# Range checks from the first load, the flag ahead of the last copies, and GpSimd's weight sums ahead of a wait

## The reference

```python
def _attn_ref(q, k, v, alpha):
    state = zeros((B, H, D, D))                      # B, H, S, D = 2, 8, 768, 48
    for t in range(S):
        state = alpha[:, :, t, :, None] * state + einsum('bhd,bhe->bhde', k[:, :, t], v[:, :, t])
        y[:, :, t] = einsum('bhd,bhde->bhe', q[:, :, t], state)
    return y

x = y as 1536 x 384
rms = sqrt(mean(x * x, axis=-1, keepdims=True) + 1e-06)
xn = x / rms * rms_g
g = xn @ w_gate                                      # 384 x 1536
x = (g / (1 + exp(-g)) * (xn @ w_val)) @ w_out
p = domain_probs / (domain_probs.sum(-1, keepdims=True) + 1e-09)
out = sum(p[:, e:e + 1] * (maximum(x @ w1[e], 0.0) @ w2[e]) for e in range(4))
```

## Time and profile before

| what | value |
|---|---|
| time, median of 3 runs | 701.38 us (701.12 to 702.0) |
| profiled execution, its own time | 698.92 us |
| its span in the profile | 697.2 us |
| PE busy | 683.6 us (98%) |
| DVE, ACT, POOL busy | 466.2, 265.3, 329.1 us |
| granted PE clock, mean | 1.0 |
| DMA moved | 35.14 MB |

### The profile page before, as it was taken

One profiled execution on the slowest core, in us unless ns is written; L12 is line 12 of the kernel. 1 busy time (PEld: TensorE's weight loads), 2 busy tenths in 40 slices (PEclk: granted clock), 3 DMA queues, 4 the chain that ended last, 5 costly groups with the idle time before them and its releaser, 6 DMA issues.

```text
span 697.2 us, 10727 instructions
## 1 busy us (share of the span) xinstructions
PE 683.6 (98%) x3989; PEld 633.9 (91%) x3989; DVE 466.2 (67%) x819; ACT 265.3 (38%) x482; POOL 329.1 (47%) x416
## 2 busy tenths in 40 slices
PE   7899999999999999999989999999999999999998
PEld 6699999999999999998979999999999999999997
DVE  6876657555556543216968777977797778767875
ACT  3932333222522243227534343433344334443430
POOL 3469761111111115770396586457645775577200
PEclk9999999999999999999999999999999999999999
DMA  8995380005102001000011100111011101100003
GB/s 183 225 182 116 98 170 0 9 1 103 35 1 77 1 2 44 3 0 24 1 46 46 47 23 24 46 46 38 9 46 45 46 2 46 46 24 1 23 1 136
DMA packets 71749, 35.14 MB, mean 50 GB/s; under 512 B 53904, under 2 KB 70672, under 8 KB 71696
## 3 DMA queue, kind: packets, MB, share of 16 engines
q1 hardware_dynamic: 71696, 34.44, 19.6%
HBM read 31.48 MB, written 2.36 MB: 49 GB/s over the span
## 4 chain that ended last, share of the span: by engine, by line
PE 88%; DVE 4%; SPq 3%; POOL 2%; ACT 1%; issue 1%; DMA 1%; DVEq 0%; POOLq 0%
PE out_ps L1370 12%; PE out_ps L1372 12%; PE out_ps L1371 12%; PE hid_ps L1363 7%; PE hid_ps L1365 6%; PE hid_ps L1364 6%; PE at_ps L1608 4%; PE at_ps L1607 4%; PE at_ps L1606 4%; PE hid_ps L1607 2%; PE hid_ps L1608 2%; PE hid_ps L1606 2%; SPq L460 2%; PE at_ps L1444 2%; PE at_ps L1458 1%; PE at_ps L1490 1%
## 5 line engine op out<-in xcount | busy, mean ns | idle before, releaser
L1249 DVE SCALAR_TENSOR_TENSOR x<-out_ps,prob,x 128x384 f32<-128x384 f32 x180 | 110.3, 613 | 58.2 <-PE out_ps L1372 58.2
L1371 PE MATMUL out_ps<-early_r,late_r 128*128 128x384 f32 x384 | 129.4, 337 | 0.0
L1370 PE MATMUL out_ps<-early_r,late_r 128*128 128x384 f32 x384 | 129.0, 336 | 0.4 <-DVE x L1249 0.4
L1372 PE MATMUL out_ps<-early_r,late_r 128*128 128x384 f32 x384 | 129.3, 337 | 0.0
L680 POOL TENSOR_TENSOR hid_lo<-act_sb,hid_hi 128x384 fp32r<-128x384 f32 x44 | 44.9, 1020 | 160.9 <-ACT hid_hi L891 160.9
L941 ACT COPY late<-at_ps 128x512 f32<-128x512 f32 x105 | 61.9, 589 | 103.8 <-PE at_ps L1608 100.8
L1215 DVE TENSOR_TENSOR act_sb<-hid_ps,act_sb 128x384 f32<-128x384 f32 x48 | 26.6, 555 | 79.6 <-PE hid_ps L1365 70.2
L1370 PEld LDWEIGHTS out_ps<-early_r,late_r 128*128 128x128 f32 x384 | 72.1, 188 | 6.6 <-DVE x L1249 0.9
L1371 PEld LDWEIGHTS out_ps<-early_r,late_r 128*128 128x128 f32 x384 | 72.0, 188 | 5.6
L1372 PEld LDWEIGHTS out_ps<-early_r,late_r 128*128 128x128 f32 x384 | 72.1, 188 | 0.0
L699 POOL TENSOR_TENSOR early<-stage 128x128 f32<-128x128 f32 x15 | 7.0, 470 | 126.4 <-PE at_ps L1608 98.8
(11 more groups left out here) (286 smaller groups left out, 1621.5 us busy)
## 6 DMA issues: line engine op xcount, KB each, us to landing
stage<-in_moe_w_dram SPq DMA_DIRECT2D x32, 384.0 KB, 3.5
alpha_all<-in_alpha_dram SPq DMA_DIRECT2D x8, 288.0 KB, 6.2
stage<-in_moe_w_out_dram SPq DMA_DIRECT2D x4, 576.0 KB, 4.0
out_dram<-x SPq DMA_DIRECT2D x12, 192.0 KB, 1.9
stage<-in_moe_w_gate_dram SPq DMA_DIRECT2D x8, 216.0 KB, 3.9
stage<-in_moe_w_val_dram SPq DMA_DIRECT2D x8, 216.0 KB, 4.0
a_tm<-in_alpha_dram SPq DMA_DIRECT2D x9, 192.0 KB, 4.2
k_tm<-in_k_dram SPq DMA_DIRECT2D x9, 192.0 KB, 3.7
```

The lines of the kernel that those rows point to most:

```text
L1249: dve.scalar_tensor_tensor(out=a, in0=part, scalar=p, in1=a, op0=ALU.mult, op1=ALU.add).then_inc(s_acc, 1)
L1370: pe.matmul(dst, ah, bh, start=first, stop=False)
L1371: pe.matmul(dst, ah, bl, start=False, stop=False)
L1372: return pe.matmul(dst, al, bh, start=False, stop=last)
```

## The change

1. Alpha is checked from other sources. The first quarter's two halves are checked from a_tm, where they are loaded for the attention anyway; only six parts are loaded to alpha_all: parts 2 and 3, the second quarter, in a new form (four runs for each partition), and parts 4 to 7, the second batch. CHECKED gives the order of the checks. As a_tm must keep its values until it has been checked, the clamped first quarter goes to a_first, which lies where woh will be; POOL's first split of an out piece waits until the transposes have read it. next_a waits for clamps and checks as well.
2. gcol's four DMAs are issued by ACT at its start instead of by SP.
3. FIRST has a new order: the checks stand earlier on ACT; y of the third pair is copied by ACT instead of DVE ("Y 2" for "YD 2"); the flag ("W") stands ahead of the last y and of its copies, and DVE reads the flag there ("ND"). The eight keep-warm matmuls of step "W" are gone. High and low parts and products of x go in the order FIRST_ORDER, in which the block copied last stands last; the square on DVE has a semaphore of its own (s_sqd); the counts that the engines wait for follow (not shown in the diff below).
4. In later quarters "SS" stands one place later.
5. sum_first of pair 2 no longer waits for s_vl and s_plain; sum_upper does.
6. In the last pair the first add_up stands ahead of the last split_bank.

```diff
@@ -96,6 +96,7 @@
         APARTS = 8
+        CHECKED = (0, 1, 4, 5, 6, 7, 2, 3)
         AW = B * H * S * D // P // APARTS
@@ -127,6 +128,10 @@
         wvl = sb("wvl", [P, KT, FF], F32R, reg_b)
+        reg_a_cl = ExitStack()
+        a_first = sb("a_first", [P, NCH, H * LANE], stack=reg_a_cl)
+        reg_a_cl.close()
+        assert NCH * H * LANE <= FT * DM
         woh = sb("woh", [P, FT, DM], F32R, reg_b)
...
@@ -398,7 +404,7 @@
         AT[STEP * NP].append(("N", 0))
-        AT.setdefault(STEP * NP + 2, []).append(("SS", 0))
+        AT.setdefault(STEP * NP + 3, []).append(("SS", 0))
         AT.setdefault(STEP * NP + 4, []).append(("R", 0))
@@ -406,12 +412,13 @@
                  (step.split() for step in ("F 10", "C 0", "T 0", "T 1", "TK 0", "TQ 0", "TK 1", "TQ 1", "F 5", "M 0",
-                                            "M 1", "S 0", "KS 0", "E 0", "C 1", "S 1", "KS 1", "T 2", "E 1", "KV 0",
-                                            "ST 0", "KV 1", "T 3", "ST 1", "E 2", "TK 2", "TQ 2", "Y 0", "TK 3",
-                                            "TQ 3", "E 3", "M 2", "M 3", "Y 1", "S 2", "KS 2", "E 4", "S 3", "KS 3",
-                                            "E 5", "KV 2", "ST 2", "KV 3", "ST 3", "E 6", "YD 2", "E 7", "SQ 1",
-                                            "YD 3", "SQ 2", "W 0", "SQD 3", "N 0", "XS 0", "SS 0", "R 0"))]
+                                            "M 1", "E 0", "S 0", "KS 0", "E 1", "C 1", "S 1", "KS 1", "E 2", "T 2",
+                                            "KV 0", "ST 0", "KV 1", "E 3", "T 3", "ST 1", "E 4", "TK 2", "TQ 2",
+                                            "Y 0", "TK 3", "TQ 3", "E 5", "M 2", "M 3", "Y 1", "S 2", "KS 2", "E 6",
+                                            "S 3", "KS 3", "E 7", "KV 2", "ST 2", "KV 3", "ST 3", "SQ 1", "Y 2",
+                                            "W 0", "SQ 2", "ND 0", "YD 3", "SQD 3", "N 0", "XS 0", "SS 0", "R 0"))]
         assert NP == 4
+        FIRST_ORDER = [PAIR_ORDER[f] for f in range(1, NP)]
@@ -486,6 +493,8 @@
                 sp.wait_ge(s_ta, NP * i)
+                sp.wait_ge(s_clamp, i + 1)
+                sp.wait_ge(s_sqa, 2)
                 load_quarter(i, 0)
@@ -499,28 +508,31 @@
             def load_alphas(c):
-                flat = alpha.rearrange("b h (x t) d -> (b h x) (t d)", x=P // BH)
-                sp.dma_start(alpha_all[:, c, :], flat[:, c * AW:(c + 1) * AW]).then_inc(s_all[c], 16)
+                if c < 4:
+                    hs = slice((c - 2) * H // 2, (c - 1) * H // 2)
+                    src = alpha[0, hs, TQ:2 * TQ, :].rearrange("h (p t) d -> p h (t d)", p=P)
+                    sp.dma_start(alpha_all[:, c - 2, :].rearrange("p (h x) -> p h x", h=H // 2), src
+                                 ).then_inc(s_all[c], 16)
+                else:
+                    flat = alpha[1].rearrange("h (x t) d -> (h x) (t d)", x=P // H)
+                    sp.dma_start(alpha_all[:, c - 2, :], flat[:, (c - 4) * AW:(c - 3) * AW]).then_inc(s_all[c], 16)
...
                 load_quarter(0, which, H // 2, H, s_half[which])
-            for which in (0, 1, 2):
-                load_quarter(0, which, 0, H // 2)
-                if which == 0:
-                    load_alphas(0)
-            load_alphas(1)
-            load_alphas(2)
-            load_quarter(0, 3, 0, H // 2)
-            load_alphas(3)
+            load_quarter(0, 0, 0, H // 2)
             load_alphas(4)
-            load_piece(0)
+            load_quarter(0, 1, 0, H // 2)
+            load_quarter(0, 2, 0, H // 2)
             load_alphas(5)
             load_alphas(6)
+            load_quarter(0, 3, 0, H // 2)
             load_alphas(7)
+            load_alphas(2)
+            load_piece(0)
+            load_alphas(3)
             load_piece(1)
-            rows_to_lanes(sp, gcol[:, :].rearrange("p (j n) -> p j n", n=1), rms_g.rearrange("(r n) -> r n", n=1),
-                          s_small, True)
             fill_holes(0)
...
@@ -688,10 +701,7 @@
                 w, u, _ = weight_sums(pair)
-                if pair == PLAIN + 1:
-                    pool.wait_ge(s_vl, len(V_SUMS))
-                    pool.wait_ge(s_plain, 6 * PLAIN)
-                elif pair > PLAIN + 1:
+                if pair > PLAIN + 1:
                     pool.wait_ge(s_mul, 15 * (pair - PLAIN - 1))
@@ -715,6 +725,9 @@
                 c, raw, done = pair % 2, raw_1(pair), 3 * (pair - PLAIN)
+                if pair == PLAIN + 1:
+                    pool.wait_ge(s_plain, 6 * PLAIN)
+                    pool.wait_ge(s_vl, len(V_SUMS))
                 pool.wait_ge(s_us, done + 3)
@@ -791,11 +804,18 @@
-                part = alpha_all[:, c, :]
+                part = alpha_all[:, (CHECKED[c] - 2) % APARTS, :]
                 if c == 0:
                     act.wait_ge(s_const, CONST_BIAS)
-                act.wait_ge(s_all[c], 16)
-                act.activation(part, part, ACT.Square, bias=consts[:, 1:2]).then_inc(s_sqa, 1)
+                if c < 2:
+                    half = slice(0, H // 2 * LANE) if c else slice(H // 2 * LANE, H * LANE)
+                    act.wait_ge(s_qka[0] if c else s_half[0], 16 * NCH)
+                    act.activation(part.rearrange("p (c h x) -> p c h x", c=NCH, x=D),
+                                   a_tm[:, :, half].rearrange("p c (h x) -> p c h x", x=LANE)[:, :, :, 0:D],
+                                   ACT.Square, bias=consts[:, 1:2]).then_inc(s_sqa, 1)
+                else:
+                    act.wait_ge(s_all[CHECKED[c]], 16)
+                    act.activation(part, part, ACT.Square, bias=consts[:, 1:2]).then_inc(s_sqa, 1)
                 act.wait_ge(s_sqa, c + 1)
@@ -803,15 +823,15 @@
+            act.wait_ge(s_const, CONST_T)
+            rows_to_lanes(act, gcol[:, :].rearrange("p (j n) -> p j n", n=1), rms_g.rearrange("(r n) -> r n", n=1),
+                          s_small, True)
             for name, i, f in events():
...
                 elif name == "SQ":
-                    if f == 2:
-                        act.wait_ge(s_yd, 2)
-                    else:
-                        act.wait_ge(s_yc, 2 * f + 2)
+                    act.wait_ge(s_yc, 2 * f + 2)
                     act.wait_ge(s_hole, 96)
...
@@ -1057,14 +1081,15 @@
-                    part = a_tm[:, :, :]
+                    part = held = a_tm[:, :, :]
                     if i == 0:
-                        part = a_tm[:, :, 0:H // 2 * LANE] if f else a_tm[:, :, H // 2 * LANE:]
+                        half = slice(0, H // 2 * LANE) if f else slice(H // 2 * LANE, H * LANE)
+                        part, held = a_tm[:, :, half], a_first[:, :, half]
                     if i == 0 and f == 0:
...
                         dve.wait_ge(s_qka[0], 16 * NCH * (i + 1))
-                    dve.tensor_scalar(part, part, MID - HALF, MID + HALF, ALU.max, ALU.min).then_inc(s_clamp, 1)
+                    dve.tensor_scalar(held, part, MID - HALF, MID + HALF, ALU.max, ALU.min).then_inc(s_clamp, 1)
                 elif name == "T":
...
@@ -1150,12 +1175,11 @@
                                           ).then_inc(s_wild, 1)
-                elif name == "N":
-                    if i == 0:
-                        dve.wait_ge(s_wild, 1)
-                        with dve.If(dve.value_load(wild[0:1, 0:1])):
-                            attention_by_steps()
-                        continue
+                elif name == "ND":
+                    dve.wait_ge(s_wild, 1)
+                    with dve.If(dve.value_load(wild[0:1, 0:1])):
+                        attention_by_steps()
+                elif name == "N" and i:
                     dve.wait_ge(s_sq, 2 * KT * (i + 1))
...
@@ -1347,8 +1371,11 @@
                     add_up(pair - 1, 11)
+                else:
+                    add_up(pair, 0)
                 split_bank("B", 0, 1)
-                add_up(pair, 0)
+                if pair < NPAIR - 1:
+                    add_up(pair, 0)
                 add_up(pair, 1)
...
@@ -1492,36 +1521,37 @@
                 elif name == "W":
-                    pe.wait_ge(s_st, NCH * NP)
-                    keep_warm(2)
                     pe.wait_ge(s_const, CONST_ALL)
...
                               ).then_inc(s_exsum, 1)
-                    keep_warm(6)
                 elif name == "SS":
...
                         pe.wait_ge(s_sqsum, i)
+                        mm = pe.matmul(at_ps[1][:, :], ones[:, :], x_nrm[:, 0, :], start=True, stop=True)
                     else:
-                        pe.wait_ge(s_sq, 2 * KT)
-                    for j in range(1 if i else KT):
-                        mm = pe.matmul(at_ps[1][:, :], ones[:, :], x_nrm[:, j, :], start=j == 0,
-                                       stop=j == (0 if i else KT - 1))
+                        for n, j in enumerate(FIRST_ORDER):
+                            if n == 0:
+                                pe.wait_ge(s_sq, 2 * KT)
```

(4 more changed lines are left out.)

36 lines of the change are left out of this document (22 added, 14 removed).

## The result

The changed kernel takes 694.44 us (694.12 to 695.21, 4 runs), the kernel before 701.25 beside it (700.11 to 702.0, 4 runs): ratio 0.9912 with an interval of 0.9891 to 0.9933. The profiled execution tells another story: 694.60 with a span of 692.9, against 698.92 and 697.2 before. That is 4.3 us less, close to the sum of 4.1. So the sum of the terms held and the step from the profiled execution to the median did not.

The account below looks back on a forecast made before the run. The prediction took TensorE (PE) as the bound, with 88% of the chain that ended last. Its terms, 1.7 + 0.2 + 1.75 + 0.45 = 4.1 us, came off the median 701.38, giving 697.3, range 695.8 to 699.3.

Parts of the forecast that it names:

- edit 4: Pair 2: POOL's sums done in its idle time remove PE's 1.84 us stop; 1.75 us gained, bounds 1.4 to 2.2.
- rival D: First stage: PE's clock falls without the keep-warm matmuls, costing 2.3 us; total gain 1.8, 699.6; chance 0.05.
- Edit 2: First stage: flag ahead of last copies, gate scaling 1.4 us earlier; with earlier loads, second val product gains 1.7.
- Edit 1: First stage: six alpha loads and gcol on ACT's queue land the x_raw fill at 30.4 instead of 32.8 us.
- Edits 3 and 5: SS one place later ends PE's wait near 102 us, 0.2; last pair's first add_up goes earlier, 0.45 us.
- B: First stage gains more: fill, clash and pieces all move by 2.4 us; total 4.8, 696.6; chance 0.13.
- C: Pair 2: another wait replaces the stop, one microsecond of 1.75 lost; total 3.1, 698.3; chance 0.08.
- F: First stage: ACT becomes the bound, fill at 31.7 or later; stage gain 0.2, total 2.6, 698.8; chance 0.09.
- E: First stage: PE's flag matmul waits for late alpha part 3; slower than before, up to 705 us; chance 0.03.
- A: First stage: weight pieces do not come earlier; stage gain 0.5 us, total 2.9, 698.5; chance 0.17.

Follow-up runs that it names:

- only_sums: The kernel before with only POOL's sums of pair 2 moved ahead of their waits; 696.88 us, ratio 0.9961.
- after_again: The changed kernel, unchanged, run once more; 694.46 us, ratio 0.9936 to the kernel before.
- gcol_on_sp_2: The changed kernel with gcol's four DMAs back on SP and ACT's constant wait ahead of them removed; 696.09 us, ratio 0.9952 to the kernel before.
- the filled version: The changed kernel with dummy matmuls in five gaps of PE in the first stage, run twice; 694.84 and 694.31 us.
- after_third: The changed kernel, unchanged, in a further series; 695.81 us, ratio 0.9942 to the kernel before.
- stop_doubled: The kernel before with four more POOL sums ahead of the eleven of pair 2, lengthening PE's stop; 702.66 us, ratio 1.0034.

## Why the prediction was wrong

**The step that failed** is the last of the sum: "the median of the runs shown is 701.38, 2.46 above it. Taking 4.1 from that: 697.3". It treats the distance of the profiled execution to the median as a constant of the program that the change leaves alone. The runs show in its place a difference between draws, and it did not come along: the changed kernel's median (694.44) is its profiled execution's own time (694.60) within 0.2.

Three parts can be told apart. About 1.5 of the 2.46 were the draw of the runs that I was shown: they lie at 701.1 to 702.0, while 94 later runs of the same kernel have a median of 699.92. Their clocks are not on record; all thirteen of the 94 that are as slow had a fall, so falls are likely there, but a slower chip can't be excluded. The other 1.0 is the distance of a profiled execution without a fall to that wider median (698.92 to 699.92). Most of it hung on the stop that edit 4 removes: a fall behind it cost 1.55 and came in three of six profiles, an estimate of 0.8 for the median, and it went with the stop. Last, the changed kernel was lucky: all its four runs have a mean clock of 1.000, where half of its 22 runs in all series (11) lie below 0.999, and the median of the 22 is 694.93. From 698.92 the same sum gives 694.8; that it comes so near to 694.44 is partly this luck. Range and chances had the same flaw as the forecast: all bounds were bounds of terms, none was for the distance, and 2.46 us is more than any of them.

**Edit 4** (the edits are numbered as in the prediction) was sized from an execution that kept its clock: 1.84 less 0.1. By the ratio of only_sums 2.7 went (1.6 to 3.8). The stop's own length is right; the 1.55 behind it, in three of six profiles, was missing, although the text named the clock as rival D, for another place. The price of the clash was nearly right: PE's first products of x, from 318.68 on, have two steps of 0.30 and 0.34 where 0.23 is usual, 0.2 in all for 0.1 forecast and up to 0.8 as its worse case.

**Edit 2** came out as worked out: fill 30.04 (30.4), low parts 33.20 (33.2), gate scaling 37.35 (37.3), second val product 55.16 (55.0). Its term of 1.7 is 1.5 by that row. The 0.2 counted for the clash is 0.22 (2.43 to 2.21); in after_again the three low parts took 1.66, so the rest of it goes in some executions.

**Edit 1** has the right sum from wrong parts. The fill was to come 2.2 earlier because SP issues earlier. gcol_on_sp_2 shows 24.39 for the issue, as early as before the change (24.49), and the fill still 2.3 earlier. That part comes from the loads ahead of it, two of alpha fewer and in another order; no run separates the two. SP's 1.7 earlier brings another 0.3 to 1.0. That gcol's issues on ACT are free is right: they end at 4.6, and the scan's root starts at 7.56 (before 7.47).

**Edits 3 and 5**: 0.65 forecast. PE's wait of 0.23 near 101 us and the 0.55 near 683 are gone in the trace. From the second val product to the last matmul PE takes 634.41 us (55.16 to 689.57) instead of 637.23, so edits 3, 4 and 5 bring 2.8 for 2.4 forecast. With the 1.5 of the first stage that is the 4.3 between the two profiled executions.

**Rivals.** B (a gain of 4.8) is nearest in its total, but not by its mechanism. C did not happen, and F not in the changed kernel; F's condition (a fill after 31.7) and E's late alpha part occurred in both profiles of the filled version. A falls: the second val product came 1.5 earlier. D's condition held (PE idle for 1.34 before 32.47) and no profile of the changed kernel has a fall there. Its price was read from the dummies of the earlier trace rows as the lower level; they take 0.23 apiece against 0.13 for the ten that start at 9.09, but the view's granted clock is 1.00 there too, so the level is read from their length alone. A fall in mid-kernel cost at most 1.57, not 2.3.

**Open.** Why the clock falls behind one stop of 1.84 us and not behind another, with no difference ahead of it that the rows show. The Trainium skill (TensorE: Matmul & The Clock Gate, Part 1) says that the window in which TensorE's activity is watched runs free and is not reset when a kernel starts, and that the point at which the clock changes therefore varies from run to run. The traces agree as far as they go: the same stop had a fall in three of six profiles. No run here tests it. Open too are what the extra 1.7 us outside the span of after_third are, why the runs that I was shown were slower than most later ones, and whether alpha part 3 and the fill are late more often with the dummies, or by chance twice.

## What to carry to other kernels

A profiled execution is one draw: compare its own time with the runs before taking its waits as the price, and where it is lower, look for what the others have and it has not. The mean granted clock of each run gives a hint of that without a trace, though a fall where PE does not bound costs little. A stop of PE costs its length and, in a part of the executions, a stretch at half clock behind it (here 1.55 us behind a stop of 1.8, in three profiles of six), so removing one can bring more than it shows, and a gain that ends at such a stop can be lost in it. Where the stop can't be removed, filling it with matmuls that nobody reads can bring the second part.

## What the runs showed of the hardware

- In nine of the profiles PE's clock went from the upper level (2.4 GHz) to the lower (1.2 GHz) for about 3.4 us (once, in stop_doubled, for 6.8): from 13.3 to 16 us on (four profiles), 27.5 (three), 32.4 (one), and behind the stop at pair 2 (four). 63 of 94 executions of the kernel before have a mean below 1.000.
- At pair 2 it fell behind the stop of 1.81 to 1.84 us in three of six profiles and behind 3.43 in the one there is, and not behind 1.00. At 32.4 it fell within an idle time of 2.10, and not at up to 1.57. But it also fell at 27.5 around an idle time of 0.98, which the kernel before has without a fall (0.97), and at 13.3 with nothing longer than 0.67 just ahead.
- The same fall cost 1.54 to 1.57 us where PE bounds (four profiles), 1.2 ahead of a chain through DVE, and little ahead of PE's gap at 17 us: the transposes behind it start at 17.63 and 18.30 with a fall, at 17.91 and 17.99 without.
- DVE's and POOL's clash is mutual: two of POOL's sums took 0.66 and 0.91 instead of 0.47 beside DVE's splits, and DVE's split of 0.56 took 0.71.
- Issuing six DMAs 1.7 us earlier on full DMA engines landed them 0.3 to 1.0 earlier; with the same issue time, 0.59 MB less ahead of them and the rest in another order, they landed 2.3 earlier (30.47 against 32.82). Both are read from few profiles: in the kernel before the squares that wait for them start anywhere from 32.0 to 33.9, and in the two profiles with dummies the early ones landed only at 32.2 and 32.5.
